# Attention and two feed-forward layers on one core: the order of VectorE's and GpSimd's steps in layer one and in the last period, and the steps of the extra operands

## The reference

```python
def reference(q, k, v, moe_w_in, moe_w_out, moe2_w_in, moe2_w_out):
    # q, k, v: (4, 8, 576, 64); block-causal attention, blocks of 64
    scores = where(block_i >= block_j, q @ k.T / 8, -1e9)
    attn = exp(scores - max); attn = attn / (sum(attn) + 1e-9)
    x = heads side by side of (attn @ v)             # (2304, 512)
    h = x @ moe_w_in                                 # (2304, 2048)
    x = (h * clip(h + 3, 0, 6) / 6) @ moe_w_out      # (2304, 512)
    h = x @ moe2_w_in
    return (h * tanh(softplus(h))) @ moe2_w_out      # (2304, 512)
```

## Time and profile before

| | |
|---|---|
| median of 3 runs | 976.23 us (974.47, 976.23, 979.89) |
| the profiled execution's own time | 974.51 us |
| its span (first to last instruction) | 972.7 us |
| instructions | 17753 |
| TensorE (matmul) busy | 98% of the span |
| VectorE, ScalarE, GpSimd busy | 74%, 69%, 42% |
| mean granted clock of TensorE | 0.998 |
| DMA | 216.43 MB, mean 223 GB/s |

### The profile page before, as it was taken

The page is one execution under the profiler, slowest core; times in us unless marked ns, Lnnn a source line. Parts: engine busy times, 40 slices in busy tenths (PEclk is TensorE's granted clock), DMA queues, the critical chain, the costliest instruction groups (busy, mean ns, idle before and its releaser), DMA issues.

```text
span 972.7 us, 17753 instructions
## 1 busy us (share of the span) xinstructions
PE 950.8 (98%) x6028; PEld 848.1 (87%) x6028; DVE 720.8 (74%) x1393; ACT 667.9 (69%) x1479; POOL 412.5 (42%) x386
## 2 busy tenths in 40 slices
PE   7999999999999999999999999999999999999998
PEld 7898888999887888889889989888988998988896
DVE  7898898786859667676757677777877777777654
ACT  7999999754445565565646567777776877776653
POOL 7899879666837577676936360000000000000000
PEclk9999999999999999999999999999999999999999
DMA  7988888658798988888765646555655654564255
GB/s 215 269 242 250 255 262 241 173 148 246 245 303 281 289 280 281 240 284 262 253 227 200 226 149 217 184 195 195 223 195 178 240 203 153 184 249 184 90 193 195
DMA packets 84602, 216.43 MB, mean 223 GB/s; under 512 B 10144, under 2 KB 16928, under 8 KB 84512
## 3 DMA queue, kind: packets, MB, share of 16 engines
q1 hardware_dynamic: 84368, 215.01, 67.4%
q10 hardware_dynamic: 144, 0.29, 0.1%
HBM read 162.07 MB, written 39.92 MB: 208 GB/s over the span
## 4 chain that ended last, share of the span: by engine, by line
PE 86%; DVE 6%; ACT 2%; POOL 2%; DMA 2%; issue 1%; SPq 0%; ACTq 0%; DVEq 0%
PE psum L1033 36%; PE psum L916 11%; PE psum L918 11%; PE psum L917 11%; PE psum L861 5%; PE psum L840 5%; PE psum L820 4%; PE psum L821 3%; DMA ext_d<-ext_made 2%; POOL xlo L1899 1%; DVE xlo L1575 1%; DVE ebuf L1640 1%; POOL osplit L1912 1%; DVE glo L1646 1%; ACT ghi L1305 0%
## 5 line engine op out<-in xcount | busy, mean ns | idle before, releaser
L1033 PE MATMUL psum<-ghi,osplit 128*128 128x512 f32 (+1 forms) x640 | 216.4, 372 | 1.3 <-POOL osplit L1912 1.3
L916 PE MATMUL psum<-xhi,whi 128*128 128x256 f32 (+1 forms) x640 | 187.8, 293 | 7.9 <-POOL xlo L1899 4.5
L918 PE MATMUL psum<-xhi,wlo 128*128 128x256 f32 (+1 forms) x640 | 187.1, 292 | 0.0
L917 PE MATMUL psum<-xlo,whi 128*128 128x256 f32 (+1 forms) x640 | 186.9, 292 | 0.0
L1033 PE MATMUL psum<-osplit,ghi 128*128 128x512 f32 x576 | 180.9, 395 | 1.1 <-DVE glo L1646 0.8
L1912 POOL TENSOR_TENSOR osplit<-oraw,osplit 128x512 fp32r<-128x512 f32 x80 | 119.1, 1492 | 119.4 <-ACT osplit L1224 119.2
L1646 DVE SCALAR_TENSOR_TENSOR glo<-ebuf,ghi 128x512 fp32r<-128x512 f32 x144 | 125.4, 871 | 30.8 <-ACT ghi L1305 22.8
L916 PEld LDWEIGHTS psum<-xhi,whi 128*128 128x128 f32 x640 | 121.3, 190 | 20.6 <-POOL xlo L1899 5.0
L1033 PEld LDWEIGHTS psum<-ghi,osplit 128*128 128x128 f32 x640 | 118.0, 189 | 17.5 <-issue 1.7
L917 PEld LDWEIGHTS psum<-xlo,whi 128*128 128x128 f32 x640 | 121.2, 189 | 10.8
L1305 ACT ACTIVATE ghi<-ebuf 128x512 fp32r<-128x512 f32 x144 | 90.0, 625 | 50.1 <-DVE ebuf L1640 31.3
(11 more groups left out here) (123 smaller groups left out, 2118.0 us busy)
## 6 DMA issues: line engine op xcount, KB each, us to landing
ext<-ext_d SPq DMA_DIRECT2D x56, 768.0 KB, 4.4
osplit<-o_d SPq DMA_DIRECT2D x80, 512.0 KB, 5.3
oraw<-in_w_out SPq DMA_DIRECT2D x80, 256.0 KB, 5.4
wraw<-in_w_in SPq DMA_DIRECT2D x26, 512.0 KB, 5.9
ext_d<-ext_made SPq DMA_DIRECT2D x32, 384.0 KB, 6.2
attn_t<-ostage SPq DMA_DIRECT2D x32, 288.0 KB, 3.9
qkin<-in_qk SPq DMA_DIRECT2D x30, 288.0 KB, 3.7
kparts<-kparts SPq DMA_DIRECT2D x30, 288.0 KB, 4.1
```

The source lines that it names most:

```text
L916: pe.matmul(dst, hi, xh, start=(start and cc == 0), stop=False, skip_group_check=True)
L917: pe.matmul(dst, hi, xl, start=False, stop=False, skip_group_check=True)
L918: last = pe.matmul(dst, lo, xh, start=False, stop=(stop and cc == 1), skip_group_check=True)
L1033: last = pe.matmul(bank(Y_BANK + c, n), stat, mov, start=(first and m == 0), stop=(final and m == 2), skip_group_check=True)
```

## The change

It has four parts. In VectorE's relu_period the two products with h and the first lower part of g come ahead of the lower parts of the extra operand and of W_out. In VectorE's mish_period the last period (s + 2 == STEPS) gets an order of its own, in which the product with h and the lower part of g of the first half come ahead of work on the second half. On GpSimd, a step now begins with the mixes of x and its first two lower parts, and ends with its adds and scales; they stood between the W_out splits. The jobs for layer two's extra operands move from odd steps 11 to 25 to even steps 12 to 26, the ahead tiles 8 to 15 the other way, from even to odd; with them the raw buffers that the two use (wraw[0] and wraw[1]) are exchanged.

```diff
--- before.py
+++ after.py
@@ -189,10 +189,10 @@
 EARLY_X_HI, EARLY_X_LO = (23, 24, 25), (24, 25, 26)
 EARLY_O_LOAD = (23, 24, 25)
 LATE_JOBS = {-1: (4, 5), 0: (6, 7)}
-EXTRA0_STEP, EXTRA1_STEP, RES1_STEP = 3, 11, LAYER - 9
-
-
-AHEAD_STEP = [2 + t if t < 8 else EXTRA1_STEP + 1 + 2 * (t - 8) for t in range(FT)]
+EXTRA0_STEP, EXTRA1_STEP, RES1_STEP = 3, 12, LAYER - 9
+
+
+AHEAD_STEP = [2 + t if t < 8 else EXTRA1_STEP - 1 + 2 * (t - 8) for t in range(FT)]
 
 
 
@@ -207,6 +207,13 @@
 SHORT_LO = {-6: ((0, 0),), -5: ((0, 1),), -4: ((0, 2),)}
 
 
+
+def next_blocks(s):
+
+    steps = [(blk, s - (FIRST_STEP[blk] - 2)) for blk in range(2, LATE_X)]
+    return [(blk, t, 0) if t < -4 else (blk, t - 4, 1) for blk, t in steps]
+
+
 def late_blocks(s):
 
     return [(blk, s - (FIRST_STEP[blk] - 2)) for blk in range(LATE_X, NBLK)]
@@ -237,7 +244,7 @@
 
 def w_slot(m):
 
-    return 0 if 2 * PAIRS <= m < 3 * PAIRS else m % 2
+    return 1 if 2 * PAIRS <= m < 3 * PAIRS else m % 2
 
 
 def w_level(m):
@@ -423,7 +430,7 @@
 
         def ahead_raw(t):
 
-            return hbuf[t % 2][:, 0:D] if t < 8 else wraw[1][:, t % 2 * D:(t % 2 + 1) * D]
+            return hbuf[t % 2][:, 0:D] if t < 8 else wraw[0][:, t % 2 * D:(t % 2 + 1) * D]
 
         def streams_before(i):
 
@@ -591,7 +598,7 @@
                     sp.wait_ge(early_lo, 2 * (m - 1))
                 elif m >= 2:
                     sp.wait_ge(w_lo, own(last_in_slot(m) + 1))
-                if m == 3 * PAIRS + 1:
+                if m == 3 * PAIRS:
                     sp.wait_ge(ahead_lo, FT)
                 cols = slice(0, RES) if half is None else slice(half * RES // 2, (half + 1) * RES // 2)
                 sp.dma_start(wraw[w_slot(m)][:, cols], w_in[layer, p, :, cols]).then_inc(w_loaded[w_slot(m)], 16)
@@ -626,7 +633,7 @@
                 if t == 0:
                     attention_stored(BATCH)
                 elif t in (8, 9):
-                    sp.wait_ge(w_lo, own(2 * PAIRS))
+                    sp.wait_ge(w_lo, own(2 * PAIRS - 1))
                 if t >= 2 and t not in (8, 9):
                     sp.wait_ge(ahead_lo, t - 1)
                 sp.dma_start(ahead_raw(t), w_out[1, t, :, :]).then_inc(ahead_loaded[t % 2], 16)
@@ -1686,11 +1693,11 @@
                 quads = quad(s + 2)
                 if first_of_block(s):
                     copy_y(BLOCK_OF[s] - 1, 3)
-                extra_jobs(s - 1)
-                ahead_os(s - 1)
                 relu6_times_h(s + 1, 0)
                 relu6_times_h(s + 1, 1)
                 split_g_lo(s + 1, 0)
+                extra_jobs(s - 1)
+                ahead_os(s - 1)
                 mixing_jobs(s)
                 if quads:
                     add_c11(s + 2)
@@ -1724,13 +1731,20 @@
                 late_x(s)
                 if quads:
                     add_c11(s + 2)
-                if now:
+                if s + 2 == STEPS:
+                    times_r(s + 1, 0)
+                    better_r(s + 1, 0)
+                    mish_times_h(s + 1, 0)
+                    times_r(s + 1, 1)
+                    split_g_lo(s + 1, 0)
+                    better_r(s + 1, 1)
+                elif now:
                     times_r(s + 1, 0)
                     better_r(s + 1, 0)
                     times_r(s + 1, 1)
                 if quads:
                     add_c12(s + 2)
-                if now:
+                if s + 2 < STEPS:
                     mish_times_h(s + 1, 0)
                     better_r(s + 1, 1)
                     split_g_lo(s + 1, 0)
@@ -1912,23 +1926,24 @@
                 nc.gpsimd.tensor_tensor(o[:, D:2 * D], raw[:, :], o[:, 0:D].bitcast(F32), ALU.subtract
                                         ).then_inc(o_lo, 1)
 
-            def next_x(s, part):
-
-                for blk in range(2, LATE_X):
-                    t, cc = s - (FIRST_STEP[blk] - 2), 0
-                    if t >= -4:
-                        t, cc = t - 4, 1
-                    if cc == 1 and KIND[blk] == SHORT:
-                        continue
+            def scale_next_x(s):
+
+                for blk, t, cc in next_blocks(s):
                     if t == -7 and blk < NBL:
-                        add_x(blk, part + 2 * cc)
-                        scale_x(blk, part + 2 * cc)
-                    if t == -6 and part == 0:
+                        for k in range(2):
+                            add_x(blk, k + 2 * cc)
+                            scale_x(blk, k + 2 * cc)
+
+            def mix_next_x(s):
+
+                for blk, t, cc in next_blocks(s):
+                    if t == -6:
                         mix_x(blk, cc)
-                    if t == -5 and KIND[blk] == SHORT:
-                        for i in range(2 * part, 2 + part):
-                            split_x_lo(blk, cc, i)
-                    elif t == -5:
+
+            def next_x_lo(s, part):
+
+                for blk, t, cc in next_blocks(s):
+                    if t == -5:
                         for i in range(2 * part, 2 * part + 2):
                             split_x_lo(blk, cc, i)
 
@@ -1947,22 +1962,26 @@
 
             for s in range(STEPS):
                 todo = [i for i in splits_at(s) if i < SPLIT_OS]
+                if s == 0:
+                    split_o(todo[0])
+                    add_x(1, 3)
+                    scale_x(1, 3)
+                    split_o(todo[1])
+                    mix_x(1, 1)
+                    for i in todo[2:]:
+                        split_o(i)
+                    continue
+                mix_next_x(s)
+                next_x_lo(s, 0)
                 for i in todo[:1]:
                     split_o(i)
-                if s == 0:
-                    add_x(1, 3)
-                    scale_x(1, 3)
                 for m in jobs_at(s):
                     if JOBS[m][0] == 1 and JOBS[m][3]:
                         mix_late(m)
-                next_x(s, 0)
-                for i in todo[1:2]:
+                next_x_lo(s, 1)
+                for i in todo[1:]:
                     split_o(i)
-                if s == 0:
-                    mix_x(1, 1)
-                next_x(s, 1)
-                for i in todo[2:]:
-                    split_o(i)
+                scale_next_x(s)
 
 
 def kernel(q, k, v, moe_w_in, moe_w_out, moe2_w_in, moe2_w_out):
```

## The result

The changed kernel takes 969.62 us in the median of 9 runs (967.34 to 974.34), the kernel before beside it 976.27 (9 runs). The ratio is 0.9936, 95% interval 0.9911 to 0.9960: faster by 0.64%, some 6.6 us, where 13.2 were forecast. 969.6 lies above the range of 961.0 to 968.5.

The account below looks back on a forecast made before the run. The prediction took TensorE, busy 950.8 of 972.7 us, as the bound, so only its idle time and clock could be won. Its terms summed to 12.0, less 0.5 for remnants: 11.5 off 974.5 gives 963.0 us, range 961.0 to 968.5.

Parts of the forecast that it names:

- A: Step 10: TensorE's wait for VectorE's product with h, behind lower parts of extra operands and W_out; 2.6 us to gain.
- T: Step 71: TensorE's wait for the last step's first glo, 0.9 us lost; 0.5 us to gain.
- (1): VectorE's new order in relu_period: claimed to take A and B, C, D to about 0, 2.6 and 1.6 us.
- My rival on A: Step 10: VectorE's order does nothing because ScalarE, behind the mixed W_in, activates h late; 2.6 us less gain, chance 0.04.
- The queue on SyncE: Later lower parts hold SyncE's loads; cost taken as 0, bounds 0 to 0.5 us in each of 8 odd steps.
- B, C, D: Steps 12, 16, 20: TensorE's product M3 waits for ScalarE's copy in hbuf; 1.6 us to gain.
- (2), (3): GpSimd's new order and the extra jobs' move to even steps: claimed to remove E, F (4.8 us) and G (0.8).
- E, F, G: Starts of steps 18, 26 and step 34: waits for GpSimd's last lower part of x; E, F 4.8 us, G 0.8.
- x still late: Rival: E and F keep about 1 to 1.5 us each and the clock stretch stays; 967 us, chance 0.13.
- GpSimd beside the first products: Rival: products slowed to 1.78 us from the step's start, so B, C, D stay; 964.6 us, chance 0.1.
- (4): Step 26: the 1.2 GHz stretch behind wait F goes with F; 1.66 us, bounds 0 and 1.66.
- (5): Last period, step 71: product and glo moved ahead shorten TensorE's wait for glo; 0.5 us, between 0 and 0.5.

Follow-up runs that it names:

- dve_old: The whole change, but with VectorE's old order in relu_period: 963.55 us, ratio 0.9869 to the kernel before.
- from10: The changed kernel, but VectorE has its new order only from step 10 on, the old one in steps 0 to 9: 963.50 us, ratio 0.9872.
- raw_first: The changed kernel, but SyncE issues a step's first two raw W_out loads ahead of load_w and load_ahead: 964.14 us, ratio 0.9879.
- dve_only: The kernel before with VectorE's new order in relu_period and nothing else of the change: 983.09 us, ratio 1.0067.
- glo_last: The changed kernel, but in relu_period only the two products precede the lower parts, g's first lower part follows them: 964.29 us, ratio 0.9883.
- x_early: The changed kernel, but in step 6 SyncE issues x's eight transfers ahead of load_w: 971.14 us, ratio 0.9946.
- act_first: The changed kernel, but ScalarE makes the extra operand's and W_out-ahead high parts one period later, behind its activation of h's second half: 967.39 us, ratio 0.9903.
- pool_order: The kernel before with GpSimd's new order and nothing else of the change: 965.16 us, ratio 0.9889.
- steps_only: The kernel before with only the steps of layer two's extra jobs and W_out ahead tiles exchanged, and their buffers: 967.40 us, ratio 0.9919.
- streams: The changed kernel with VectorE's old relu_period order, and the third- and fourth-last W_out tiles fetched into ext: 963.09 us, ratio 0.9868.
- tail_old: The changed kernel with VectorE's old order in relu_period and the old last period too: 963.49 us, ratio 0.9870.
- dve_old_again: The changed kernel with VectorE's old relu_period order, measured once more beside two others on one chip: 964.48 us, ratio 0.9884.

## Why the prediction was right, and where it failed

**The direction and most of the terms were right; the gain was put down to the wrong edit.** By the table above each of B to G came within 0.2 us, and 11.66 of the 12.0 are to be had (dve_old). From step 0 on the changed kernel is 4.5 us short of the 11.5: A is 3.1 short (-0.47 for 2.6), steps 4, 5 and 13 cost 1.4 that I had at 0, T is 0.6 short, and the rest came 0.6 better than forecast.

**(1) VectorE's order: the step that failed.** "mixing_jobs starts where it did, because the same instructions precede it." The same instructions do precede it, but they don't end when they did. Two of them, the products and glo, wait for ScalarE and TensorE; the two lower parts wait for nothing much, and in the old order they ran in front of those waits. Put behind them they come on top: glo ended at 311.6 and 3.8 us of lower parts followed. In before the mixes of step 9 began 4.90 us into the step (306.11 - 301.21), in after 10.3 (315.21 - 304.90). My rival on A named the mechanism, ScalarE behind the mixed W_in, and I gave it 0.04 on the strength of that sentence. Over the kernels with the two products in front in step 10 the idle time follows the start of ScalarE's activation, counted from the start of step 10:

| | activation | idle |
|---|---|---|
| from10 | -1.19 | 0 |
| raw_first | -0.27 | 0 |
| dve_only | 1.53 | 1.30 |
| glo_last | 1.60 | 1.47 |
| after | 3.01 | 2.87 |
| x_early | 3.30 | 3.16 |

The idle time is 0.13 to 0.23 less than the activation's delay in all four that wait. act_first takes the activation out of that place, and the 0.84 left is the queue on VectorE.

**The queue on SyncE, taken at 0.** I had named it the dear one, and worked its cover out for step 15 alone. It acts in steps 3 to 9, where the mixes make the round closed: ScalarE's activation, VectorE's product, glo, lower parts, mixes, ScalarE's high part, the next activation; with it, lower part, load_ahead, load_o, ScalarE. Three edits, each at another link of it, shorten step 10's wait: to 0.84 (act_first), 1.47 (glo_last) and 0 (raw_first). The lateness cost 0.73 + 0.52 + 0.19 in steps 4, 5 and 13, and kept A. That the order is harmless from step 10 on (from10) shows that my estimate held where I made it.

**A, cured by another part.** I priced A as 0.96 + 1.77 in front of the product. The size is right, but 1.77 is a part that takes 0.68 while GpSimd is idle, and the stack stood late because two mixes took 1.40 each for the same reason. GpSimd's order moves its two-input work off that stretch (pool_order). That a part is slow beside another engine was in the earlier trace rows; I used it only as a price of the products, not as a cause of A.

**B, C, D** went (1.80), but not by my reason alone. VectorE's new order by itself clears steps 12 and 20 (dve_only), and so does the exchange of the steps by itself (steps_only); GpSimd's order by itself clears none (pool_order), and step 16 is clear only where the exchange and GpSimd's order are both there. All three go in dve_old without VectorE's new order, so that order is not needed for them.

**(2), (3) E, F, G were right in size and in reason.** GpSimd's chain for block 3, in order of time (first add, last lower parts):

```profile
377.73 1.30 POOL L1876 TENSOR_TENSOR xst<-xst 128x512 f32<-128x512 f32 x1
...
397.48 3.27 POOL L1913 TENSOR_TENSOR xlo<-xst,xhi 128x512 fp32r<-128x512 f32 x2
```

From the first add to the last lower part 23.0 us, for 23.4 reckoned; the block starts at 403.05, 2.3 us behind that end, for 0.8 reckoned. The first add also came earlier, 5.94 us into step 15 for 7.15 before. "x still late" did not happen. Either edit would have done for most of it: GpSimd's order alone clears E, F and G, the exchange alone E and all but 0.5 of F.

**GpSimd beside the first products.** The condition came, the price did not. In step 16 of after:

```profile
382.31 1.78 DVE L1647 SCALAR_TENSOR_TENSOR ebuf<-ebuf,hbuf 128x512 f32<-128x512 f32 x1
```

The first product takes 1.78 beside GpSimd, as in the earlier trace rows, and no matmul waits. The rule weighed in the prediction (the Trainium skill, SBUF — State Buffer, Who interferes with whom) holds for the durations: 0.42 or 1.40 for one mix, 0.68 or 1.77 for one lower part. It spoke against the change where it cost nothing, and would have explained A.

**(4) The clock: right, 1.66.** No stretch at 1.2 GHz lies ahead of the last matmuls in after. The runs of after lie 7.0 us apart, though, not closer than those of before (7.1); without the wait of step 10 it is 1.6 in dve_old and 1.2 in pool_order, but 5.1 in from10, so I can't tell it to that wait.

**(5) The last period: mis-sized, 0.5 taken, nothing measured in the changed kernel (-0.09).** Steps 70 and 71 of after, TensorE's waits in order of time; beside the earlier trace rows:

```profile
956.11 0.70 PE L1040 MATMUL psum<-osplit,ghi 128*128 128x512 f32 x2 [0.30 <-DMA osplit<-o_d]
...
958.01 0.73 PE L1040 MATMUL psum<-osplit,ghi 128*128 128x512 f32 x2 [0.28 <-DVE glo L1653]
...
959.99 0.70 PE L1040 MATMUL psum<-osplit,ghi 128*128 128x512 f32 x2 [0.33 <-DMA osplit<-o_d]
```

The wait for glo fell from 0.78 to 0.28, as forecast. But TensorE, 0.5 earlier, now meets a W_out tile that isn't there (0.33 at 959.99). streams bears that out: with these tiles early, the 0.5 stays. It also stays in glo_last, which has the old slots but no wait for a tile in step 71 (15.76 for the two steps), so in one kernel the size of this term hangs on when the transfers land.

**What stays open.** The waits of steps 0 to 3 differ by up to 1.1 us between kernels that are alike there (step 1 takes 12.88 in tail_old, 13.97 in dve_old_again), and I did not look for the cause. raw_first on top of dve_old was not run.

## What to carry to other kernels

"The same instructions stand in front" says when a step starts only if none of them waits for another engine: an instruction that needs nothing is free in front of a waiting one and can cost its whole length behind it, so for each moved instruction ask what wait it used to fill. Where the engines wait for each other in a round, follow a delay once around it, in the steps with the most work in the round and not in the one that is easiest to read. And when a change has several parts, run each alone: here one part alone gave 9.6 us and another cost 4.7.

## What the runs showed of the hardware

- One VectorE instruction with two inputs in SBUF takes 0.42 or 1.40 us (mix, 128x256), 0.96 or 2.06 (extra part, 128x768), 0.68 or 1.78 (W_out part, 128x512), the low figure with GpSimd idle, the high one only beside GpSimd's work; values in between occur there too (0.84 for a mix, 1.23 for a W_out part). Moving GpSimd's work in time (pool_order) removed a 2.4 us wait of TensorE for VectorE, which I had not expected.
- The granted clock. A stretch at 1.2 GHz came behind the waits of 3.97 and 3.98 us in dve_only, behind that of 3.16 in x_early (the window below, around its end, columns as in the earlier trace rows) and behind wait F of before, about 2.2. In dve_old_again one came in the attention, right behind a wait of 1.82 us at 111.08 (second window). None came behind the 2.87 in after, nor behind A (2.43) and E of before. So the length of the one wait does not tell whether a stretch follows.

```profile
319.40:323.00 3.60, 3.56 (x16) 3.27 (x17) 3.20 (x5) 0.72 (x2) 1.17 (x1) 0.61 0.99 323
```

```profile
111.20:114.70 3.50, 3.50 (x15) 3.33 (x16) 1.28 (x5) 1.74 (x4) 0.86 (x2) 0.51 0.95 303
```
